# Top-32 attention with two feed-forward layers: the mask on ScalarE by a steep leaky rectifier, the later normalising on GpSimd

## The reference

```python
scores = scale * np.matmul(q, k.transpose(0, 1, 3, 2))
kth = np.partition(scores, -top_k, axis=-1)[..., -top_k:-top_k + 1]
scores = np.where(scores >= kth, scores, -1000000000.0)
attn = np.exp(scores - np.max(scores, axis=-1, keepdims=True))
attn = attn / (np.sum(attn, axis=-1, keepdims=True) + 1e-09)
x = np.matmul(attn, v)                 # as 2304 tokens x 512
h = x @ w_in;  x = np.maximum(0.01 * h, h) @ w_out               # 512 -> 2048 -> 512
h = x @ w_in2; g = np.where(h >= 1, h, np.where(h <= -1, 0, (h + 1) ** 2 / 4)); out = g @ w_out2
```

## Time and profile before

| | |
|---|---|
| median of three runs | 1202.42 us (1201.8 to 1202.47) |
| the profiled execution | 1198.35 us, its span 1196.4 us |
| PE, weight loads | 1108.2 us busy (93%), 999.2 us (84%) |
| DVE | 924.3 us (77%) |
| ACT | 701.0 us (59%) |
| POOL | 608.7 us (51%) |
| the chain that ended last | PE 71%, DVE 19%, POOL 3%, issue 3%, ACT 3%, DMA 1% |

### The profile page before, as it was taken

The page is one execution under the profiler, slowest core; times in us unless marked ns, Lnnn a source line. Parts: engine busy times, 40 slices in busy tenths (PEclk is TensorE's granted clock), DMA queues, the critical chain, the costliest instruction groups (busy, mean ns, idle before and its releaser), DMA issues.

```text
span 1196.4 us, 21062 instructions
## 1 busy us (share of the span) xinstructions
PE 1108.2 (93%) x7360; PEld 999.2 (84%) x7360; DVE 924.3 (77%) x2088; ACT 701.0 (59%) x1579; POOL 608.7 (51%) x582
## 2 busy tenths in 40 slices
PE   3547998899999999999999989999899999999998
PEld 2335887778989988889987978998789999999998
DVE  7999999989799998998989999969989006300234
ACT  5676878756577765666666756566775424312232
POOL 5676778835366643655536744346644323222222
PEclk9758999989999999999999999999999999999999
DMA  6789997766667787767666756455356677787764
GB/s 228 280 300 342 348 346 285 270 229 206 220 223 233 255 285 257 275 230 258 236 233 211 249 182 222 159 198 175 121 194 217 201 256 250 252 283 251 250 239 150
DMA packets 86792, 287.12 MB, mean 240 GB/s; under 512 B 9632, under 2 KB 13472, under 8 KB 86688
## 3 DMA queue, kind: packets, MB, share of 16 engines
q1 hardware_dynamic: 79200, 270.04, 65.5%
q10 hardware_dynamic: 7488, 15.73, 3.9%
HBM read 247.46 MB, written 38.27 MB: 239 GB/s over the span
## 4 chain that ended last, share of the span: by engine, by line
PE 71%; DVE 19%; POOL 3%; issue 3%; ACT 3%; DMA 1%; POOLq 0%; SPq 0%; ACTq 0%
PE ps_f L812 19%; PE ps_f L820 19%; PE ps_f L813 18%; DVE top L1067 7%; DVE work L1070 7%; PE ps_av L771 6%; PE ps_s L727 3%; PE ps_t L748 2%; DVE drop L1076 2%; PE ps_t L727 2%; DVE part_r L1094 2%; PE ps_t L754 2%; POOL gate L644 1%; POOL drop L630 1%; POOL part_o L650 1%
## 5 line engine op out<-in xcount | busy, mean ns | idle before, releaser
L1067 DVE MAX8 top<-work 128x8 f32<-128x576 f32 x432 | 309.3, 742 | 0.1
L812 PE MATMUL ps_f<-xy,w_ring 128*128 128x384 f32 (+2 forms) x896 | 288.8, 322 | 4.5 <-ACT xy L994 2.5
L820 PE MATMUL ps_f<-gate,w_ring 128*128 128x384 f32 (+2 forms) x896 | 281.3, 314 | 9.5 <-POOL gate L644 9.4
L812 PE MATMUL ps_f<-gate,w_ring 128*128 128x384 f32 (+2 forms) x896 | 286.0, 319 | 1.0 <-ACT part_o L975 0.6
L630 POOL TENSOR_TENSOR drop<-scores,drop 128x576 f32<-128x576 f32 x144 | 207.9, 1444 | 150.1 <-DVE drop L1076 150.1
L820 PE MATMUL ps_f<-xy,w_ring 128*128 128x384 f32 (+2 forms) x896 | 280.8, 313 | 1.8 <-POOL xy L654 1.6
L813 PE MATMUL ps_f<-xy,w_ring 128*128 128x384 f32 (+2 forms) x896 | 280.1, 313 | 0.0
L813 PE MATMUL ps_f<-gate,w_ring 128*128 128x384 f32 (+2 forms) x896 | 280.0, 312 | 0.0
L1070 DVE MATCH_REPLACE8 work<-top,work 128x576 f32<-128x576 f32 x288 | 212.7, 739 | 0.0
L812 PEld LDWEIGHTS ps_f<-xy,w_ring 128*128 128x128 f32 x896 | 169.7, 189 | 20.5 <-issue 9.3
L644 POOL TENSOR_TENSOR gate<-part_r,gate 128x384 fp32r<-128x384 f32 (+2 forms) x112 | 101.5, 909 | 157.4 <-ACT gate L979 157.2
(11 more groups left out here) (83 smaller groups left out, 1822.0 us busy)
## 6 DMA issues: line engine op xcount, KB each, us to landing
w_ring<-w_split SPq DMA_DIRECT2D x412, 512.0 KB, 4.2
w_split<-w_ring SPq DMA_DIRECT2D x36, 512.0 KB, 6.0
raw<-wd SPq DMA_DIRECT2D x64, 256.0 KB, 4.3
w_split<-xy SPq DMA_DIRECT2D x28, 512.0 KB, 3.7
kq<-kqd ACTq DMA_DIRECT2D x12, 576.0 KB, 5.8
v_sb<-vd ACTq DMA_DIRECT2D x12, 320.0 KB, 3.2
out_t<-y_acc ACTq DMA_DIRECT2D x12, 192.0 KB, 3.6
kq<-kqd SPq DMA_DIRECT2D x3, 576.0 KB, 6.7
```

Source lines behind the costliest of these rows:

```text
L812: pe.matmul(out, w[:, 0, m], high, start=first, stop=False)
L820: mm = pe.matmul(out, w[:, 0, m], low, start=False, stop=end)
L1067: dve.max(top[:, t % T_SLOTS, 8 * r:8 * r + 8], source(t, r)).then_inc(dve_step, 1)
```

## The change

DVE no longer writes a mask. `find_bounds` writes two columns per row: minus the 32nd largest score times SCALE, and the difference of the 32nd and the largest, times SCALE. ACT applies a leaky rectifier (`Prelu`) with slope 1e30 below zero to SCALE times the score less the threshold (`keep`), into `probs`: what is below the threshold becomes hugely negative, the rest stays. Then it takes the exponential in place, with the second column as its bias. `neg_max`, `drop`, POOL's `mask` and the waits for them are gone: copying scores needs no wait any more, since `keep` stands ahead of it on ACT. For the 8 items of the first chunk (16 tiles) ACT still normalises; for the other 72 (128 tiles) POOL does, by `tensor_scalar` in place, in the same step as ACT did.

```diff
-            def mask(t):
-                it = ITEM_OF[t]
-                pool.wait_ge(dropped, t + 1)
-                slot = drop[:, t % D_SLOTS, :]
-                pool.tensor_tensor(slot, scores[:, it.n % S_SLOTS, t - it.first, :], slot, ALU.add).then_inc(masked, 1)
+            def normalise(it):
+                pool.wait_ge(inv_ready, it.n + 1)
+                for a in range(it.tiles):
+                    p = probs[:, it.n % P_SLOTS, a * S:(a + 1) * S]
+                    op = pool.tensor_scalar(p, p, row_inv[:, it.n % T_SLOTS, a:a + 1], None, ALU.mult)
+                op.then_inc(probs_ready_late, 1)
...
-                if READY[0] <= s < TILES + MASK_LAG:
-                    mask(s - MASK_LAG)
+                if s + 1 in OUT_AT and not starts_early(OUT_AT[s + 1].gp):
+                    normalise(OUT_AT[s + 1])
...
             def copy_scores(it):
-                if it.n >= S_SLOTS:
-                    act.wait_ge(masked, ITEMS[it.n - S_SLOTS].last + 1)
...
+            def keep(t):
+                it = ITEM_OF[t]
+                a = t - it.first
+                act.wait_ge(bounds_ready, t + 1)
+                need(act, transposed, it.n - P_SLOTS + 1)
+                act.activation(probs[:, it.n % P_SLOTS, a * S:(a + 1) * S], scores[:, it.n % S_SLOTS, a, :], ACT.Prelu,
+                               bias=bounds[:, t % 8, 0:1], scale=SCALE, alpha=STEEP).then_inc(kept, 1)
+
             def exponential(t):
-                act.wait_ge(neg_max_ready, t + 1)
-                act.wait_ge(masked, t + 1)
-                need(act, transposed, it.n - P_SLOTS + 1)
-                act.activation(probs[:, it.n % P_SLOTS, a * S:(a + 1) * S], drop[:, t % D_SLOTS, :], ACT.Exp,
-                               bias=neg_max[:, t % 8:t % 8 + 1], scale=SCALE,
+                act.wait_ge(kept, t + 1)
+                p = probs[:, it.n % P_SLOTS, a * S:(a + 1) * S]
+                act.activation(p, p, ACT.Exp, bias=bounds[:, t % 8, 1:2],
                                accum_out=row_sum[:, it.n % T_SLOTS, a:a + 1]).then_inc(exp_done, 1)
...
                 elif s < TILES + EXP_LAG:
-                    exponential(s - EXP_LAG)
+                    keep(s - EXP_LAG)
                 for u in first:
                     event(u)
                 if s == READY[0]:
                     exponential(s - 1 - EXP_LAG)
+                elif s < TILES + EXP_LAG:
+                    exponential(s - EXP_LAG)
...
-                if s + 1 in OUT_AT:
-                    normalise(OUT_AT[s + 1])
...
-            def find_drop(t):
-                need(dve, exp_done, t - D_SLOTS + 1)
-                dve.tensor_scalar(drop[:, t % D_SLOTS, :], scores[:, it.n % S_SLOTS, t - it.first, :],
-                                  top[:, t % T_SLOTS, TOP_K - 1:TOP_K], DROPPED, ALU.is_lt,
-                                  ALU.mult).then_inc(dropped, 1)
+            def find_bounds(t):
+                first, last = top[:, t % T_SLOTS, 0:1], top[:, t % T_SLOTS, TOP_K - 1:TOP_K]
+                dve.tensor_scalar(bounds[:, t % 8, 0:1], last, -SCALE, None, ALU.mult)
+                dve.tensor_scalar(bounds[:, t % 8, 1:2], last, first, SCALE, ALU.subtract,
+                                  ALU.mult).then_inc(bounds_ready, 1)
```

More of the change, by code:

```diff
@@ L399, in scores_first @@
     return s in OUT_AT
+SCALED_EARLY = sum(starts_early(it.gp) for it in ITEMS)
 SCORED_EARLY = sum(score_step(it) < READY[0] - 1 for it in ITEMS)
@@ L431, in build @@
         top = sb("top", [P, T_SLOTS, TOP_K])
-        neg_max = sb("neg_max", [P, 8])
-        drop = sb("drop", [P, D_SLOTS, S])
+        bounds = sb("bounds", [P, 8, 2])
         probs = sb("probs", [P, P_SLOTS, 2 * S])
@@ L1033, in _ @@
                     copy_values(CHUNKS[0].last_gp)
+                    keep(s - 1 - EXP_LAG)
                 elif s < TILES + EXP_LAG:
-                    exponential(s - EXP_LAG)
+                    keep(s - EXP_LAG)
                 for u in first:
@@ L1042, in _ @@
                         copy_scores(it)
-                if s + 1 in OUT_AT:
-                    normalise(OUT_AT[s + 1])
                 for u in second:
                     event(u)
+                if s == READY[0]:
+                    keep(s - EXP_LAG)
                 if s in VALUES_AT:
@@ L1112, in finish_first @@
                 dve.wait_ge(dve_step, count + 3)
-                find_drop(t - 1)
+                find_bounds(t - 1)
                 dve.wait_ge(scores_copied, 2 * ITEM_OF[t].n + 2)
@@ L1116, in finish_first @@
                 dve.wait_ge(dve_step, count + 4)
-                dve.tensor_scalar(neg_max[:, t % 8:t % 8 + 1], top[:, t % T_SLOTS, 0:1], -SCALE, None,
-                                  ALU.mult).then_inc(neg_max_ready, 1)
                 drop8(t, 0)
```

19 lines of the change are left out of this document (9 added, 10 removed).

## The result

The changed kernel took 1193.77 us (median; 1191.66 to 1196.05, four runs) against 1202.11 us (1201.74 to 1202.47, four runs): a ratio of 0.9938 with a 95% interval of 0.9918 to 0.9958. It is faster by 0.6%. The forecast was 1183 us, so the sign and the range (1172 to 1198) held, but of the 19 us forecast only 8 came, less than half.

The account below looks back on a forecast made before the run. The prediction took DVE to bound the start-up and 32.9 us of PE gaps to be the gain available until 920 us. It summed -6 and -13 to -19 us, giving 1183 us on the median, range 1172 to 1198.

Parts of the forecast that it names:

- DVE in the start-up: Until 98 us, dropping find_drop and neg_max shortens each of 16 DVE steps by 0.38 us: -6.1 us (-3.5 at the dear end).
- the pair of bounds: Two new one-column DVE operations per tile, taken at 0.10 us together, with 0.26 as the upper bound.
- ACT and the weights in the start-up: ACT gains a keep per tile (0.67 us) yet does not limit; its 1.3 us wait for raw before each second weight piece goes.
- rival 1: ACT or the weight loads set the start-up: 1199 us if the 1.3 us wait stays, 1189 if halved; chance 0.13.
- POOL's multiplication: 128 tensor_scalar normalisings on POOL, taken at 1.0 us each (0.51 to 1.44): 128 us in place of 208 us of masks.
- POOL has its time to spare: At 1.0 us per multiplication POOL already has slack, so a cheaper 0.5 to 0.6 us would not move the sum.
- Rival 3: POOL's two multiplications before a gate delay join and low half; decides from about 1.5 us each: +17, 1213 us; chance 0.07.
- The common part, -13: From 98 to 920 us, somewhat over half of 23.2 us of PE gaps goes: -13 us, bounds 5 and 25.
- the four stretches named: 98 to 120, 200 to 250, 600 to 720 and 800 to 860 us, whose PE gaps were expected to shrink.
- DVE and POOL at their port: Shared-port blocking lengthens DVE operations; without find_drop and with POOL 80 us lighter, fewer such meetings were expected.
- the 0.38 us: Saving per DVE step, 0.43 + 0.05 - 0.10, counted as at least that in the common part too.
- Clock in 200 to 250: In that window PE was to work over 45 of 50 us at a granted clock of 1.0, up from 0.90.

Follow-up runs that it names:

- e6: e1 plus a mask-shaped addition per tile on POOL, result unread, with copying of scores waiting for it again: 1197.8 us, ratio 0.9949.
- e1: Changed kernel, but ACT normalises all 80 items and POOL neither masks nor multiplies: 1182.3 us, ratio 0.9844 against the kernel before.
- e3: Changed kernel with an item's two POOL multiplications taken apart, the second behind the second third of the step's units: 1190.6 us, ratio 0.9915.
- e5: e1 plus the old comparison back on DVE for every tile, its result read by nobody: 1203.8 us, ratio 1.0010 against the kernel before.
- e4: Changed kernel with POOL's tensor_scalar replaced by tensor_tensor, its second input the column repeated over 576: 1187.9 us, ratio 0.9886.
- e0_again: The changed kernel itself, unaltered, measured and profiled a second time: 1194.2 us, ratio 0.9920 against the kernel before.

## Why the prediction was right in part and wrong in size

- **DVE in the start-up: right.** The step went from 5.38 to 5.07 us and the first product from 97.6 to 92.3 us: -5.3 against -6.1. The term that was too low is the pair of bounds, 0.19 us between starts and not 0.10, within the bounds given (0.05 to 0.26): 16 x 0.09 is 1.4 us, more than the 0.8 that are missing, so that the rest of the start-up gave a little more than forecast.
- **ACT and the weights in the start-up: right, against rival 1.** The wait before the second piece is gone, and the reason given for it stands (e6). `keep` to exponential took 0.79 us between starts; no wait came of it.
- **POOL's multiplication: the step that failed.** "The same engine, same shape, with two tensors read is 1.44 us and is the upper bound" and "I take 1.0, as it reads one tensor and not two" were both wrong. It takes 1.747 us (1.715 at least), and with a second tensor, of a repeated column, 1.19. The count of tensors read says nothing of the price of this operation on POOL, so that 1.44 bounded nothing. From it followed "POOL has its time to spare" and "against: POOL's whole load falls"; both fell with it, and the sum had no term for what the multiplications hold up. In its place the runs show 9 to 11 us given back (e1), through joins that come late and hold the copying of scores on ACT and so PE's transposes. The Trainium skill that was cited there (GPSIMD Engine Reference, Engine selection: roughly line-rate with one input) gave an estimate of 0.5 to 0.6 us; the measurement is three times that and decides.
- **Rival 3: its cause came, by another path and in another size.** The bound at which it decides was "about 1.5 us for one multiplication", and this was passed. Its sign on PE did not come: the wait for POOL's gate was to be above 15 us and fell to 4.9. PE waits before the transposes instead, in four places for 9.5 us in place of three for 4.9, and ACT 14 us more for joins. It gave back 9 to 11 us by e1, not the 17 of its sum; and what it gave back was not all that the masks freed, since this was there after all. Whether it takes a pair in one go stays open (e3).
- **The common part, -13: right for the masks, wrong for the change.** e1 shows -18.8 in all, -13.2 of it behind the first product. The places were right too: of the 12.1 us of idle time that PE lost in e1, 10.0 stood in the four stretches named. The size, "somewhat over half" of the gaps, was a guess that came out well. Half of the change was priced right and the other half taken for free.
- **DVE and POOL at their port**: the gain was put into the 0.38 us as "part of why". e5 shows operations of DVE made longer beside POOL's, by 5.8 us in the start-up alone, and only where POOL has no wait that keeps it away. The Trainium skill (SBUF — State Buffer, SBUF: two separate sides) has a shared port pair under an exclusive lock. The comparison at 38.92, with 1.60 us instead of 0.50, agrees; so does the square at 192.44 in the chain above, 1.46 us beside POOL's `w_ring` and 0.41 at 195.28.
- **Clock in 200 to 250: wrong.** Forecast 1.0 with PE over 45 of 50; it was 0.85 with 44.0, and 0.90 with 43.8 in e1.

Open: what makes the clock fall. In the kernel before it stays at 1.00 through gaps of 0.56 and 2.00 us at 701 to 704, and falls behind gaps of 0.51 and 1.41 in the changed one. It falls in e3 too (0.74 in 700 to 720) and in e4 elsewhere. `e0_again` shows that 6 of the 16.8 us come and go with the same gaps; whether the multiplications have a part in the rest isn't shown. Open too: whether POOL's load as such or its blocks in front of joins cost the 9 to 11 us, since every run changed both together.

## What to carry to other kernels

When work moves to an engine with no row for the operation, a row of another operation on the same shape is not a bound: leave the upper end open, and ask what is queued behind it there. A wait in an engine's queue can be useful by keeping it apart from another engine's operations that it would lengthen; in e5, with the wait gone and the comparisons kept, these took 12.1 us instead of 8.4. And an engine with half its time idle can be the wrong place for work, if its queue holds the short joins on which everybody waits: here ACT, busy for 77% of the common part in e1 (636 us of 822), carried the multiplications better than POOL, busy for 60% of it with them (493 us).

## What was not expected of the hardware

- POOL on 128x576 f32: `tensor_scalar` with a column as its scalar 1.75 us; `tensor_tensor` with that column repeated 1.19 us, with one tensor read twice 1.17 us (e6), with two different tensors 1.44 us. On 128x8 the `tensor_scalar` takes 0.31 us.
- A DVE operation on two columns took 0.87 us instead of 0.16 beside a POOL operation (e5, 38.14).
- Four transposes took 1.06 us in place of 0.60 for some microseconds behind a gap of 1.41 us, where a longer gap in the same place (2.00 us, kernel before) had left the clock at its full level; the same kernel with the same gaps lost 16.8 us to the clock in one execution and 10.6 in another.
